# Routed experts: the second projection moves the high and low columns in one matmul, and the first projection has four PSUM banks

## What is computed

```python
N, D, E, F = (1152, 512, 8, 1024)
logits = x @ w_gate
expert_idx = np.argmax(logits, axis=1)
for e in range(E):
    mask = expert_idx == e
    xe = x[mask]
    h = np.maximum(xe @ w1[e], 0.0)
    ye = h @ w2[e]
    out[mask] = gate_w[mask, None] * ye
```

## Time and profile before

| | before |
|---|---|
| time, median of 3 runs | 772.53 us (771.75 to 774.69) |
| the profiled execution: time / span | 771.7 / 769.9 us |
| mean granted TensorE clock | 0.986 |
| TensorE matmul busy | 733.8 us, 95% of the span |
| VectorE / ScalarE / GpSimd busy | 307.5 / 263.9 / 154.3 us |
| routed stage, first matmul of line 1085 to first of the dense stage | 170.78 to 361.24 us |

### The profile page before, as it was taken

The page is one execution under the profiler, slowest core; times in us unless marked ns, Lnnn a source line. Parts: engine busy times, 40 slices in busy tenths (PEclk is TensorE's granted clock), DMA queues, the critical chain, the costliest instruction groups (busy, mean ns, idle before and its releaser), DMA issues.

```text
span 769.9 us, 14486 instructions
## 1 busy us (share of the span) xinstructions
PE 733.8 (95%) x5044; PEld 664.1 (86%) x5045; DVE 307.5 (40%) x804; ACT 263.9 (34%) x632; POOL 154.3 (20%) x174
## 2 busy tenths in 40 slices
PE   6989999789999999998999999999999999999996
PEld 5777777579999999998999989999999999999995
DVE  4787777505545455544431324312144121212211
ACT  2777776105545445553321113211132111111110
POOL 4666566131221221221110001100001000001001
PEclk9899999899999999999999999999999999999998
DMA  7735513146656677654420003300030000001001
GB/s 185 218 93 156 162 29 108 49 147 191 192 183 183 192 210 215 192 191 145 138 82 1 1 1 107 113 0 0 0 82 27 0 0 0 0 0 41 14 27 41
DMA packets 56054, 71.46 MB, mean 93 GB/s; under 512 B 33968, under 2 KB 33968, under 8 KB 55504
## 3 DMA queue, kind: packets, MB, share of 16 engines
q1 hardware_dynamic: 54384, 65.01, 28.8%
q0 software_dynamic: 1456, 4.76, 1.7%
q10 hardware_dynamic: 176, 1.22, 0.4%
HBM read 65.78 MB, written 5.19 MB: 92 GB/s over the span
## 4 chain that ended last, share of the span: by engine, by line
PE 88%; issue 3%; SPq 2%; DVE 2%; DMA 1%; POOL 1%; DVEq 1%; ACT 1%; ACTq 0%
PE bank L1134 26%; PE wide L1145 26%; PE wide L1097 11%; PE bank L1085 9%; PE bank L1021 4%; PE bank L1003 3%; PE wide L955 3%; PE bank L986 1%; POOL x_slots L472 1%; PE wide L960 1%; PE bank L1066 1%; PE wide L929 1%; DMA stages<-in_moe_w 1%; SPq L288 1%; DVEq L848 1%
## 5 line engine op out<-in xcount | busy, mean ns | idle before, releaser
L1134 PE MATMUL bank<-x2Th,w_hi 128*128 128x384 f32 (+1 forms) x384 | 129.2, 337 | 2.0 <-DVE x2Tl L840 2.0
L1134 PE MATMUL bank<-x2Tl,w_hi 128*128 128x384 f32 (+1 forms) x384 | 129.4, 337 | 0.0
L1134 PE MATMUL bank<-x2Th,w_lo 128*128 128x384 f32 (+1 forms) x384 | 128.9, 336 | 0.0
L481 POOL TENSOR_TENSOR w_lo<-stages,w_hi 128x1024 fp32r<-128x1024 f32 x22 | 52.5, 2388 | 380.4 <-ACT w_hi L606 380.4
L1085 PE MATMUL bank<-xT,w_hi 128*128 128x192 f32 x512 | 96.5, 280 | 6.0 <-DVE h1T L832 3.7
L1097 PE MATMUL wide<-h1T,w_hi 128*128 128x192 f32 x512 | 94.2, 275 | 0.0
L606 ACT ACTIVATE w_hi<-stages 128x1024 fp32r<-128x1024 f32 x88 | 92.7, 1053 | 0.0
L824 DVE TENSOR_TENSOR w_lo<-stages,w_hi 128x1024 fp32r<-128x1024 f32 x66 | 80.8, 1224 | 23.7 <-ACT w_hi L606 23.4
L1085 PEld LDWEIGHTS bank<-xT,w_hi 128*128 128x128 f32 x512 | 83.2, 195 | 7.8 <-DVE h1T L832 4.8
L638 ACT ACTIVATE h_0h<-bank 128x384 fp32r<-128x384 f32 x48 | 23.6, 492 | 188.3 <-PE bank L1134 188.3
L873 DVE SCALAR_TENSOR_TENSOR h_0l<-bank,h_0h 128x384 fp32r<-128x384 f32 x48 | 26.8, 558 | 141.1 <-ACT h_0h L638 141.1
(11 more groups left out here) (164 smaller groups left out, 1248.9 us busy)
## 6 DMA issues: line engine op xcount, KB each, us to landing
stages<-in_moe_w SPq DMA_DIRECT2D x96, 512.0 KB, 4.1
cum_bc<-cum_dram SPq DMA_DIRECT2D x3, 1152.0 KB, 9.3
x_rows<-x_slots SPq DMA_DIRECT2D x9, 256.0 KB, 2.9
q_nat<-in_q SPq DMA_DIRECT2D x16, 128.0 KB, 2.6
k_nat<-in_k SPq DMA_DIRECT2D x16, 128.0 KB, 3.7
v_nat<-in_v SPq DMA_DIRECT2D x16, 128.0 KB, 2.6
cum_bc<-cum_dram ACTq DMA_DIRECT2D x1, 1152.0 KB, 8.0
x_rows<-x_slots SPq DMA_DIRECT2D x9, 128.0 KB, 3.0
```

The costliest lines, as they stand in the source:

```text
L481: g.tensor_tensor(w_lo[par][:, c], stage[3][:, :], w_hi[par][:, c].bitcast(F32), ALU.subtract).then_inc(lo_done[3], 1)
L1134: last = te.matmul(bank[ft % 2][:, 0:CHUNK], w1_of((w_hi, w_lo)[st][par], kk, ft * P, P), x_mv, start=(n == 0), stop=(n == 11))
```

## The change

`down` issues for each output part one matmul with w_hi whose moving operand is the high and the low columns side by side (2 x 192 = 384), and one with w_lo and the high columns (192). The first fills 384 columns of the bank: columns 0 to 191 hold the sum for the high part, 192 to 383 that for the low part. After the tile VectorE adds the two halves with a tensor_reduce into a new SBUF tensor `y1`, one for each `wide` tensor, and counts `x2_sum`; the high and low parts of the output are taken from `y1`, and `down(0)` of the next tile waits for `x2_sum` instead of `x2_lo`. `up_bank` goes round four banks, so `up(ft)` waits for the low part of step ft-4. `turn_x` uses banks 0 and 1 and waits for the low part of step 5. VectorE's `split_lo` of piece 0, 1, 2, 4, 5, 6 stands one step later.

```diff
@@ -50,6 +50,7 @@
 SLOTS = N + TOK
 MAXT = N // TOK
 LAG = 3
+UP_BANKS = 4
 XROW = 520
 GATE, PROB, TOKEN = DM, DM + 1, DM + 1 + 4
 SCALE = 1.0 / 8.0
@@ -148,6 +149,7 @@
             x_rows = sb("x_rows", [P, 2, DM], F32, b)
             xT = sb("xT", [P, KD, 2, TOK], F32R, b)
             h1T = sb("h1T", [P, LAG + 1, 2, TOK], F32R, b)
+            y1 = sb("y1", [P, KD, TOK], F32, b)
 
         acc = sb("acc", [P, N // P, DM], F32)
         h2 = [[sb(f"h2_{i}{c}", [P, CHUNK], F32R) for c in "hl"] for i in range(2)]
@@ -161,7 +163,7 @@
             qk_hi qk_lo bias_ready scores_ready max_ready exp_done turned_act turned_dve pT_act pT_dve
             values_ready oT_ready out_turned sums_eps_ready inv_ready norm_done sums_cleared zeros_ready
             slots_zeroed wg_loaded r_step ex_done onehot_ready rank_ready route_ready scattered payload_in
-            hi_done x_rows_loaded xT_psum xT_hi xT_lo h1_psum h1_hi h1_lo x2_psum x2_hi x2_lo
+            hi_done x_rows_loaded xT_psum xT_hi xT_lo h1_psum h1_hi h1_lo x2_psum x2_sum x2_hi x2_lo
             h2_psum h2_hi h2_lo y2_ready y2_added acc_cleared p2_loaded p2_step token_ready out_stored passed
             pads_zeroed""".split()
         m = {n: sem(n) for n in names}
@@ -196,13 +198,14 @@
 
 
         def up_bank(ft):
-            return bank[ft % 2][:, 0:TOK]
+            return bank[ft % UP_BANKS][:, 0:TOK]
 
         def down_bank(dt):
-            return half[dt][:, 0:TOK]
+            return half[dt][:, 0:2 * TOK]
 
         def down_pair(pr):
-            return wide[pr][:, :].rearrange("p (a k) -> p a k", a=2)[:, :, 0:TOK]
+            banks = wide[pr][:, :].rearrange("p (c k) -> p c k", c=2)[:, :, 0:2 * TOK]
+            return banks.rearrange("p c (a k) -> p c k a", a=2)
 
         TURN_ROWS = (P, TOK - P)
 
@@ -210,7 +213,7 @@
             return nc.s_assert_within(off + j * TOK, 0, N, skip_runtime_bounds_check_because="a tile that is run starts at a row of its expert")
 
         def turn_bank(g):
-            return bank[2 + g][:, 0:KD * TURN_ROWS[g]].rearrange("p (c r) -> p c r", c=KD)
+            return bank[g][:, 0:KD * TURN_ROWS[g]].rearrange("p (c r) -> p c r", c=KD)
 
         def xT_part(hl, g):
             return xT[:, :, hl, g * P:g * P + TURN_ROWS[g]]
@@ -617,8 +620,8 @@
                 if split is not None:
                     split_hi(*split, KF - 1)
                 for pr in range(2):
-                    act.wait_ge(m["x2_psum"], t * 2 + (pr + 1))
-                    sc.activation(x2T_part(0, pr, col), down_pair(pr), ACT.Copy).then_inc(m["x2_hi"], 1)
+                    act.wait_ge(m["x2_sum"], t * 2 + (pr + 3))
+                    sc.activation(x2T_part(0, pr, col), y1[:, 2 * pr:2 * pr + 2, :], ACT.Copy).then_inc(m["x2_hi"], 1)
                 act.reg_add(T, T, 1)
 
             with act.Fori(0, E1 // 2) as pair:
@@ -814,8 +817,8 @@
                     ve.tensor_tensor(xT_part(1, g), turn_bank(g), xT_part(0, g).bitcast(F32),
                                      ALU.subtract).then_inc(m["xT_lo"], 1)
 
-            dve.sem_inc(m["h1_lo"], 2)
-            dve.sem_inc(m["x2_lo"], 2)
+            dve.sem_inc(m["h1_lo"], UP_BANKS)
+            dve.sem_inc(m["x2_sum"], 2)
             x_lo(0)
 
             def split_lo(ge, par, u):
@@ -832,12 +835,15 @@
                     ve.scalar_tensor_tensor(out=h1T[:, ft % (LAG + 1), 1, :], in0=up_bank(ft), scalar=0.0,
                                             in1=h1T[:, ft % (LAG + 1), 0, :].bitcast(F32), op0=ALU.max,
                                             op1=ALU.subtract).then_inc(m["h1_lo"], 1)
-                    if split is not None and ft % 4 < 3:
-                        split_lo(*split, ft)
+                    if split is not None and ft > 0 and (ft - 1) % 4 < 3:
+                        split_lo(*split, ft - 1)
                 x_lo(t + 1)
                 for pr in range(2):
+                    dve.wait_ge(m["x2_psum"], t * 2 + (pr + 1))
+                    ve.tensor_reduce(y1[:, 2 * pr:2 * pr + 2, :], down_pair(pr), AX.X, ALU.add).then_inc(m["x2_sum"], 1)
+                for pr in range(2):
                     dve.wait_ge(m["x2_hi"], t * 2 + (pr + 1))
-                    ve.tensor_tensor(x2T_part(1, pr, col), down_pair(pr), x2T_part(0, pr, col).bitcast(F32),
+                    ve.tensor_tensor(x2T_part(1, pr, col), y1[:, 2 * pr:2 * pr + 2, :], x2T_part(0, pr, col).bitcast(F32),
                                      ALU.subtract).then_inc(m["x2_lo"], 1)
                 dve.reg_add(T, T, 1)
 
@@ -1089,13 +1095,15 @@
                 def down(f):
                     if e is not None and f % 2 == 0:
                         pe.wait_ge(lo_done[f // 2], e * 2 + 2)
-                    pe.wait_ge(m["h1_lo"], t * KF + (f + 3))
+                    pe.wait_ge(m["h1_lo"], t * KF + (f + 1 + UP_BANKS))
                     if f == 0:
-                        pe.wait_ge(m["x2_lo"], t * 2 + 2)
+                        pe.wait_ge(m["x2_sum"], t * 2 + 2)
                     for dt in range(KD):
-                        for n, (st, mv) in enumerate(PASSES):
-                            last = te.matmul(down_bank(dt), w2_of((w_hi, w_lo)[st][par], f)[:, dt * P:(dt + 1) * P], h1T[:, f % (LAG + 1), mv, :],
-                                             start=(f == 0 and n == 0), stop=(f == KF - 1 and n == 2))
+                        w_rows = [w2_of(w[par], f)[:, dt * P:(dt + 1) * P] for w in (w_hi, w_lo)]
+                        te.matmul(down_bank(dt), w_rows[0], h1T[:, f % (LAG + 1), :, :].rearrange("p a k -> p (a k)"),
+                                  start=(f == 0), stop=False, skip_group_check=True)
+                        last = te.matmul(down_bank(dt)[:, 0:TOK], w_rows[1], h1T[:, f % (LAG + 1), 0, :],
+                                         start=False, stop=(f == KF - 1), skip_group_check=True)
                         if f == KF - 1 and dt % 2 == 1:
                             last.then_inc(m["x2_psum"], 1)
 
@@ -1103,6 +1111,7 @@
                     up(ft)
                     if ft >= LAG:
                         down(ft - LAG)
+                pe.wait_ge(m["h1_lo"], t * KF + (KF - UP_BANKS + len(TURN_ROWS) + UP_BANKS))
                 turn_x(t + 1)
                 for f in range(KF - LAG, KF):
                     down(f)
@@ -1120,7 +1129,7 @@
                                 tile(par)
 
             done = pe.snap(T, min_val=E1, max_val=E1 + MAXT)
-            pe.wait_ge(m["x2_lo"], done * 2 + 2)
+            pe.wait_ge(m["x2_lo"], done * 2)
             alone(pe)
 
             def dense_chunk(e, c, par):
```

## The result

The changed kernel took **767.17 us** (765.18 to 767.92, 5 runs) against 772.38 (771.75 to 774.69, 5 runs) of the kernel before on the same chip: ratio 0.992, 95% interval 0.991 to 0.994. It is faster by 0.8%, where I had said 1.6%, and 0.2 us above the range. The profiled execution took 767.17 us, its span 765.4.

What follows compares the result with a forecast made beforehand. TensorE's own stream, busy 95% of the span, was taken as the bound, with one weight load per routed matmul. −12.2 − 4.8 + 2.4 + 2.4 = −12.2 us from 771.7 gave 759.5, stated as 760; range 752 to 767.

Steps and rivals of the forecast that it cites:

- pairs of matmuls: Second projection `down`: a 384- and a 192-column matmul take 287.5 ns against 335.1 for three; −12.2 us over 64 steps.
- waits for low halves: First projection `up`: four banks remove TensorE's seven waits for VectorE's low halves, −4.8 us; other end 0.
- `down(0)` at tile changes: Routed tile changes: VectorE's sums make the first low half late for `down(0)`, +2.4 us; 0 with sums of 0.96 us.
- start of the dense stage: End of the routed stage: the last low part is done later, +2.4 us; +1.2 with the short sum.
- Nothing else on the path changes: Rest of the kernel: no further effect on the path, the dense stage being the same code.
- my signs of being wrong: On TensorE: a short matmul behind a long one costing other than 112 ns, or a wait standing in no row.
- rival 1: `down`: weight loads go further ahead than one matmul, a pair costs 269 ns, 4.7 us more gained, 755; chance 0.13.
- The sums: VectorE: two TENSOR_REDUCE a tile, 768 inputs from PSUM, 1.55 us each; other end 0.96 us.
- rival 4: Tile changes: VectorE's sums make `down(0)` wait at each; 0.5% slower at 2.5 us a sum, near 776; chance 0.04.
- ScalarE's waits for DMA: ScalarE at weight piece 4: it waits about 3 us for the later refill, covered by the 6 us of slack.
- Rival 3: Weight feed: later splits delay the four stages' refills, a tile can't go under today's, time near 772; chance 0.07.
- Rival 2: First projection: waits for low halves stay because VectorE carries 3.1 us more a tile; 4.8 us more, 765; chance 0.15.

Runs made afterwards that it cites:

- banks alone: Kernel before without TensorE's code for further tiles, plus only four banks, transposes in banks 0 and 1 and the weight split one step later: 764.31 us, 0.990.
- the 144 instructions: Changed kernel with the 80 warm-up matmuls written out without a loop, 144 more instructions ahead of the routed loop: 755.07 us, 0.978.
- 250 more: Changed kernel with one whole block, about 250 instructions, more ahead of the loop: 763.34 us, 0.988.
- the last kernel: Changed kernel with 144 more instructions ahead of the loop and 13 unused 512-column matmuls ahead of the dense stage: 752.60 us, 0.974.
- The kernel with two banks: Kernel before without TensorE's code for further tiles, plus only the second projection's pairs and VectorE's sums; also called the pair alone: 783.15 us, 1.013.
- the short kernel before: Kernel before with TensorE's code for an expert's second and further tiles left out: 772.18 us, 1.000.
- the short kernel: Changed kernel with TensorE's code for an expert's second and further tiles left out: 754.40 us, 0.977.
- 64 instructions more: Changed kernel with the warm-up loop as 2 times 40 matmuls, 64 more instructions ahead of the routed loop: 765.79 us, 0.993.

## Why the prediction was wrong

The sum, step by step; the measured sizes are in us against before.

| step | predicted | measured | from |
|---|---|---|---|
| pairs of matmuls | −12.2 | −12.8 | pitch of the banks alone 22.44, of the whole change 20.84: 1.60 × 8 |
| waits for low halves | −4.8 | −8.2 | banks alone 764.31 against 772.51 |
| `down(0)` at tile changes | +2.4 | 0 | no such wait |
| start of the dense stage | +2.4 | +2.9 | wait 2.0 to 3.3, and 1.6 of lower clock |
| "Nothing else on the path changes" | 0 | +12.8 | branch: 767.17 against 754.40 |

**The step that failed** is the last sentence of the sum: "Nothing else on the path changes; the dense stage is the same code." Without it the result is 754.4, 0.977; with it the gain shrinks to a third. The change takes 32 matmuls out of each of the loop's four copies of a tile, some 250 instructions of TensorE's code in all. That moves what lies where, and two branches of the first pass took 4 us. A wait of TensorE that stands in no row was among my signs of being wrong. The trace of before had the sign, and I put it in the earlier trace rows and read past it: at 195.67 TensorE started "0.57 late" by "issue", which I used as cover for a tile change. Its branch took 1.10 us there, the second 0.33 and the six others 0.21. That the fetch of code is behind it is shown by the loops that don't stay loaded, with their packets; for the two branches of the first pass it rests on the duration, on the 144 instructions that take it away, and on the packets beside them. It isn't settled which positions wait: I found no count by blocks that fits the branches of all kernels, the second wait fails to appear at 250 more, and the last kernel shows its one in one execution of five. The kernel with 144 more fetches as many packets in its first pass (five between 187 and 214 us, after five between 191 and 226) and doesn't wait. A fetch that is at times just early enough would do it; that was only argued.

**The pair** came out in its sum: 287.5 ns foreseen, 285 to 290 measured from pair to pair, so rival 1 (269 ns) is out as a number. The parts did not come out: the starts lie 0.20 and 0.09 us apart rather than 0.176 and 0.112, and I had named a short matmul that costs other than 112 ns as a sign of being wrong. That the load of the short matmul hides and the next one doesn't is thus an argument that the total fits; no run here shows it.

**The waits for low halves** were the gain foreseen, mis-sized: −8.2 for −4.8. I had corrected one wait from 0.22 to 0.38 and scaled that to seven; with four banks the pitch fell from 23.45 us (mean of the seven that go behind the first) to 22.44, 1.0 us a tile. I had scaled from the smallest of the seven waits. At the longest (222.56) the view has 0.92, and the start lies 1.19 us behind the one ahead of it, 1.08 over the pace. What makes up the rest I haven't traced.

**The sums** I took at 1.55 us by the earlier trace rows and kept 0.96 as the other end; 0.95 it is. This read from PSUM, 192 elements apart, took what the slope of the copies gave; the row of 1296 ns for 640 inputs in steps of 8 was no guide to it. The Trainium skill (VectorE: DVE Perf Modes, The TRN2 errata — SBUF-src ops pay a fixed extra latency per instruction) has a formula for an fp32 tensor_tensor add, (N+151)/0.96 ns. Carried over to these 768 inputs it gives an estimate of 0.96 us, which agrees with the 0.95. With the short sum my own working gave nothing lost at tile changes, and so it was. The kernel with two banks shows that the mechanism of rival 4 is real; it lacked four `up`s of room rather than a slower sum.

**The start of the dense stage**: by the short sum I had +1.2, and the wait grew by 1.3. That the taken sum of 1.55 us gave +2.4 is luck: the other 1.6 us came from the granted clock behind a wait of 3.3 us, which I hadn't costed. In the profiled execution of the kernel before the clock stays at 1.00 behind 2.0 us. It doesn't always: the short kernel before waits 1.95 us there and has this behind it (granted clock 0.66).

```profile
360.00:365.00 5.00, 4.05 (x15) 4.08 (x16) 1.34 (x7) 0.31 (x1) 0.00 (x0) 0.66 0.25 92
```

**ScalarE's waits for DMA** came (15.2 us in 13 places, the longest 1.8, where I had foreseen about 3 at piece 4 of each tile) and don't reach TensorE: its waits of the short kernel name none. Rival 3 is out. Rival 2 is too: no wait for a low half was left.

That the 760 lies within 8 us of the result is luck: two errors of opposite sign. The terms of the sum took off 6 us too little (754.4 without the waits for code), and the term that was missing is 12.8.

## What to carry to other kernels

A change to an unrolled kernel also moves its code, and on TensorE with a runtime loop that can cost more than the change gives: 16 instructions made a kernel 4.6% slower. Where a gain falls short, look for waits by "issue" and at the records of branches before looking at the work, and try the same kernel with a few instructions written out elsewhere. Where two parts of a change share a cover, as the sums and the banks do here, cost each without the other too.

## What the runs showed of the hardware

- A loop of some 1,700 instructions on TensorE ran from loaded code in its later passes (branches 208 to 213 ns, 4 code packets in 205 us, none of them in the later passes), and with 16 instructions more ahead of it it didn't (branches 1.3 to 3.8 us, 30 packets, 34 us slower). With 144 more it was 53 us slower, with about 250 more back within 3.5 us. The Trainium skill (Runtime: NRT & Kernel Launch, Instruction fetch mechanics) speaks of a purely sequential prefetch without a cache; the later passes here show code that stays.
- A taken branch took 0.21 us in the later passes of a loop that stayed loaded, 0.33 to 1.4 us in some first passes, and 3.3 to 4.6 us at its longest. Each long one in the first pass of the changed kernel lengthened its tile by 3.0 us (no fall of the clock) to 6.4 us (with it).
- The granted clock was 0.50 for about 6 us behind waits of 3.1 us in after, and 1.00 behind one of 2.7 with 64 instructions more. It also fell behind some waits of 1.7 us (the pair alone) and one of 1.95 (the short kernel before), and not behind 2.0 in the kernel before: in these traces the length of the wait alone doesn't tell.
- Matmuls of fp32 in one pass: 192 columns 111.7 ns, 384 columns 175.8, one of each in turn 285 to 290 together.
